# Retention and two feed-forward layers on one core: up products by Strassen's algorithm on pairs of token chunks, k and v rows of the longer prologue on ACT's DMA queue

## The reference

```python
for t in range(S):
    state = gamma * state + einsum('bhd,bhe->bhde', k[:, :, t], v[:, :, t])
    y[:, :, t] = scale * einsum('bhd,bhde->bhe', q[:, :, t], state)   # gamma[h] = 1 - 2^(-5-h)
x = y as (3072, 512)
h = x @ w_in;   g = h * cos(h);                       x = g @ w_out   # 512 -> 2048 -> 512
h = x @ w2_in;  g = where(h >= 1, h, where(h <= -1, 0, (h + 1)**2 / 4));  out = g @ w2_out
```

## Time and profile before

| what | value |
|---|---|
| median of 3 runs | 1165.73 us (1165.51 to 1165.99) |
| span of the profiled execution | 1163.8 us |
| granted TensorE clock, mean | 0.997 |
| PE busy | 1151.9 us, 99% |
| PE weight loads busy | 943.1 us, 81% |
| DVE / ACT / POOL busy | 556.8 / 380.4 / 132.4 us |
| instructions | 14906 |
| DMA | 74.57 MB, mean 64 GB/s |

### The profile page before, as it was taken

The page is one execution under the profiler, slowest core; times in us unless marked ns, Lnnn a source line. Parts: engine busy times, 40 slices in busy tenths (PEclk is TensorE's granted clock), DMA queues, the critical chain, the costliest instruction groups (busy, mean ns, idle before and its releaser), DMA issues.

```text
span 1163.8 us, 14906 instructions
## 1 busy us (share of the span) xinstructions
PE 1151.9 (99%) x5892; PEld 943.1 (81%) x5892; DVE 556.8 (48%) x836; ACT 380.4 (33%) x606; POOL 132.4 (11%) x113
## 2 busy tenths in 40 slices
PE   7999999999999999999999999999999999999998
PEld 5888888888888888788788888888888888888887
DVE  5555555556556555555554433433433433433433
ACT  2444332333333333323555322222222222222222
POOL 4445011001001010100354000000000000000000
PEclk8999999999999999999999999999999999999999
DMA  6433212022113112220452301001101001000100
GB/s 230 160 111 128 73 54 74 19 102 63 37 35 112 44 48 91 73 73 1 145 172 64 145 1 73 37 1 73 37 1 73 36 0 72 36 0 0 37 1 37
DMA packets 35481, 74.57 MB, mean 64 GB/s; under 512 B 3936, under 2 KB 4064, under 8 KB 33888
## 3 DMA queue, kind: packets, MB, share of 16 engines
q1 hardware_dynamic: 35424, 73.75, 18.7%
HBM read 54.86 MB, written 18.87 MB: 63 GB/s over the span
## 4 chain that ended last, share of the span: by engine, by line
PE 97%; DMA 1%; DVE 1%; SPq 0%; ACT 0%; issue 0%; DVEq 0%
PE up L378 45%; PE acc L401 23%; PE acc L403 22%; PE att L339 2%; PE att L318 2%; PE att L335 2%; PE att L359 1%; DMA raw<-in_w1u 0%; DMA q_sb<-in_q_t 0%; DVE x_lo L532 0%; PE acc L318 0%; PE att L354 0%; DVE am L471 0%; DVE x_lo L481 0%; DVE q_sb L461 0%
## 5 line engine op out<-in xcount | busy, mean ns | idle before, releaser
L378 PE MATMUL up<-x_hi,wu_hi 128*128 128x512 f32 x768 | 299.6, 390 | 1.1 <-DVE g_raw L514 1.1
L378 PE MATMUL up<-x_lo,wu_hi 128*128 128x512 f32 x768 | 298.8, 389 | 0.0
L378 PE MATMUL up<-x_hi,wu_lo 128*128 128x512 f32 x768 | 298.8, 389 | 0.0
L523 DVE SCALAR_TENSOR_TENSOR g_lo<-g_raw,g_hi 128x512 fp32r<-128x512 f32 x192 | 137.3, 715 | 181.9 <-ACT g_hi L608 181.9
L608 ACT ACTIVATE g_hi<-g_raw 128x512 fp32r<-128x512 f32 x192 | 121.3, 632 | 192.7 <-PE acc L403 108.8
L378 PEld LDWEIGHTS up<-x_hi,wu_hi 128*128 128x128 f32 x768 | 144.1, 188 | 32.8 <-DVE g_raw L514 2.5
L378 PEld LDWEIGHTS up<-x_hi,wu_lo 128*128 128x128 f32 x768 | 144.1, 188 | 30.0
L378 PEld LDWEIGHTS up<-x_lo,wu_hi 128*128 128x128 f32 x768 | 144.2, 188 | 29.7
L401 PE MATMUL acc<-g_hi,wd_hi 128*128 128x512 f32 x384 | 156.1, 406 | 0.0
L401 PE MATMUL acc<-g_hi,wd_lo 128*128 128x512 f32 x384 | 150.1, 391 | 0.0
L401 PE MATMUL acc<-g_lo,wd_hi 128*128 128x512 f32 x384 | 149.9, 390 | 0.0
(11 more groups left out here) (57 smaller groups left out, 899.5 us busy)
## 6 DMA issues: line engine op xcount, KB each, us to landing
q_sb<-in_q_t SPq DMA_DIRECT2D x24, 256.0 KB, 4.0
k_sb<-in_k_t SPq DMA_DIRECT2D x24, 256.0 KB, 4.0
x_hi_scratch<-x_hi SPq DMA_DIRECT2D x24, 256.0 KB, 3.0
x_lo_scratch<-x_lo SPq DMA_DIRECT2D x24, 256.0 KB, 3.4
x_hi<-x_hi_scratch SPq DMA_DIRECT2D x6, 1024.0 KB, 4.8
x_lo<-x_lo_scratch SPq DMA_DIRECT2D x6, 1024.0 KB, 6.9
kn<-in_k_n SPq DMA_DIRECT2D x22, 256.0 KB, 2.9
v_sb<-in_v_n SPq DMA_DIRECT2D x20, 256.0 KB, 2.6
```

The source lines that it names most:

```text
L378: last = nc.tensor.matmul(up[j % 2][:, :], w[:, j, k, :], x[:, par, k, :], start=(k == 0 and x is x_hi and w is wu_hi), stop=(k == KT - 1 ...
L523: nc.vector.scalar_tensor_tensor(out=g_lo[:, s, :], in0=g, scalar=2.0 if layer == 1 else 1.0, in1=g_hi[:, s, :].bitcast(F32), op0=ALU.mult ...
```

## The change

The up product of layer and chunk becomes one of a pair of chunks. X is cut into X11, X12 (k tiles 0, 1 and 2, 3 of the first chunk) and X21, X22 (the same of the second), W into four quarters by k half and by f half, and with Winograd's form of Strassen's algorithm seven products of half the depth take the place of eight. A quad q is the f tiles q and q + 8 of both chunks: its W quarters are 128 wide, it gives H11, H12, H21, H22. Three of four up banks hold the products of a quad; P6, P7 and P4 are added up in one bank, P1 and P2 in another, P5 and P3 in the third, and DVE adds what is between (`sum_u2`, `sum_u3`, `sum_h22`, `sum_h21`, `sum_h12`) from PSUM and SBUF.

A span is a pair of chunks in a layer: six spans of eight quads, then a tail. Down products of the first chunk of the pair go beside the quads (one of tile q - 1 behind P6, one of q - 1 + 8 behind P5), those of the second chunk's 16 tiles after the quads in the tail, 18 in all with the last two of the first. Their gates wait in SBUF (`late`).

Raw weights of up products are loaded again in each span, a quad at a time into two buffers; POOL makes four sums of 128 columns for each k tile (`t_sums`), ACT the high half of all seven blocks in one instruction of 896 columns (`t_high`), POOL the low half (`t_low`). The sums of X are made by POOL (512 columns, 8 a span), the splits of the 14 operand tiles by ACT and DVE. In layer 1 the multiplication with 1/(2 pi) goes from DVE to ACT (`turns`).

The prologue has eight units of retention, with all q, k, v and row-form k of them in buffers of their own but one; SP issues q and k, ACT issues the rows of k and v of units 0 to 6 as its first instructions. The other sixteen units lie in the tails of spans 0 and 1, in one block each of outputs, outer products and the scores of the next unit, with one down product (two behind the last but one) between blocks. The last four units have no outer products. Layer 1's result is stored and read as one float32 tensor. All loops over chunks are written out. Down results leave PSUM by copies on ACT (`rows_first`, `rows_second`), except the last two of the program, on DVE.

```diff
-        def walk(eng, body):
...
-                    elif (layer, place) != (2, "last"):
-                        up_product(blk + 1, 1 - par, layer, "middle", j + LEAD - FT)
-                    if not opening:
-                        retention(blk, layer, place, j)
-                    down_product(blk, layer, place, j)
...
-                dve.wait_ge(up_done, n + 1)
-                if layer == 1:
-                    nc.vector.tensor_scalar(g.bitcast(I32), h, TURNS, None, ALU.mult).then_inc(turns_done, 1)
...
+PRODUCTS = ["p1", "p6", "p2", "p7", "p5", "p4", "p3"]
+BLOCK = {"p1": 0, "p7": 1, "p2": 2, "p3": 3, "p5": 4, "p6": 5, "p4": 6}
+W11, W12, W21, W22, T1, T2, T4 = range(7)
...
+SPLITS = [("p1", 0, X11), ("p1", 1, X11 + 1), ("p2", 0, X12), ("p2", 1, X12 + 1), ("p7", 0, X11), ("p7", 1, X11 + 1),
+          ("p4", 0, X22), ("p6", 0, SUM2), ("p5", 0, X21), ("p3", 0, X12),
+          ("p4", 1, X22 + 1), ("p6", 1, SUM2 + 1), ("p5", 1, X21 + 1), ("p3", 1, X12 + 1)]
+NS = len(SPLITS)
+SUMS_BEFORE = {4: 1, 5: 2, 7: 3, 8: 4, 9: 5, 11: 6, 12: 7, 13: 8}
+NSUM = 8
...
+DOWN = [(1, f) for q in range(QUADS - 1) for f in (q, q + QUADS)]
+LATE = [f for q in range(QUADS) for f in (q, q + QUADS)]
+TAIL = [(1, QUADS - 1), (2, LATE[0]), (2, LATE[1]), (1, FT - 1)] + [(2, f) for f in LATE[2:]]
+DOWN += TAIL
+ND = len(DOWN)
...
+        def quad_banks(s, q):
+            return [up_banks(s)[(3 * q + i) % 4] for i in range(3)]
+        def unit_banks(u):
+            if u < AHEAD:
+                return banks[0:4] if u % 2 == 0 else banks[4:8]
+            return early_banks(u // AHEAD - 1)
...
+            def load_rows(u):
+                first = u < AHEAD
+                if not first and u % AHEAD >= 1:
+                    sp.wait_ge(y_done, u)
+                    sp.wait_ge(outer_done, min(u, UNITS - KT))
+                sp.dma_start(unit_kn(u), heads(k_n[u])).then_inc(kn_in_first[u] if first else kn_in, 16)
+                sp.dma_start(unit_v(u), heads(v_n[u])).then_inc(v_in_first[u] if first else v_in, 16)
+            def load_raw(n):
+                layer, q = n // (QUADS * PAIRS), n % QUADS
+                if n >= 2:
+                    sp.wait_ge(product_done["p3"], n - 1)
+                if n % QUADS == 1 and n // QUADS in (1, 2):
+                    sp.wait_ge(y_done, AHEAD * (n // QUADS + 1))
+                    sp.wait_ge(outer_done, min(AHEAD * (n // QUADS + 1), UNITS - KT))
+                for kt in range(2):
+                    sp.dma_start(raw[n % 2][:, kt, 1, 0:4, :], up_input[layer][q, kt]).then_inc(raw_in[n % 2][kt], 16)
...
+            for s in range(SPANS):
+                for q in range(QUADS):
+                    n = QUADS * s + q + 1
+                    if n < QUADS * SPANS:
+                        load_raw(n)
+                    if q == 0 and s:
+                        store_rows(s - 1, 2)
+                    if s == 0 and q + 1 < QUADS:
+                        load_wd(0, q + 1)
+                u = AHEAD * (s + 1)
+                if s < PAIRS - 1:
+                    load_columns(u)
+                    load_rows(u)
+                    load_columns(u + 1)
+                elif s + 1 < SPANS:
+                    load_x2(s + 1, 0)
+                store_rows(s, 1)
+                if s < PAIRS - 1:
+                    load_rows(u + 1)
+                    for i in range(2, AHEAD):
+                        load_columns(u + i)
+                        load_rows(u + i)
+                elif s + 1 < SPANS:
+                    load_x2(s + 1, 1)
+                if s == PAIRS - 1:
+                    for q in range(QUADS):
+                        load_wd(1, q)
...
+            def product(s, q, name):
+                n = QUADS * s + q
+                i = BLOCK[name]
+                bank_1, bank_2, bank_3 = quad_banks(s, q)
+                to = {"p1": bank_1, "p2": bank_1, "p6": bank_2, "p7": bank_2, "p4": bank_2,
+                      "p5": bank_3, "p3": bank_3}[name]
+                if q == 0:
+                    pe.wait_ge(xlo_done, NS * s + max(m for m in range(NS) if SPLITS[m][0] == name) + 1)
+                if name == "p1" and q >= 2:
+                    pe.wait_ge(h12_done, n - 1)
+                if name == "p6" and q >= 1:
+                    pe.wait_ge(g_done, 4 * (n - 1) + 1)
+                if name == "p5" and q >= 1:
+                    pe.wait_ge(h21_done, n)
+                if name == "p2":
+                    pe.wait_ge(p1_copied, n + 1)
+                if name == "p7":
+                    pe.wait_ge(u2_done, n + 1)
+                if name == "p4":
+                    pe.wait_ge(u3_done, n + 1)
+                if name == "p3":
+                    pe.wait_ge(h22_done, n + 1)
+                w = tw[n % 2]
+                for kt in range(2):
+                    if name == "p1":
+                        pe.wait_ge(tlo_done, 2 * n + kt + 1)
+                    opens = name in ("p1", "p6", "p5") and kt == 0
+                    nc.tensor.matmul(to[:, :], w[:, kt, 0, i, :], x_hi[:, i, kt, :], start=opens, stop=False,
+                                     skip_group_check=True)
+                    nc.tensor.matmul(to[:, :], w[:, kt, 0, i, :], x_lo[:, i, kt, :], start=False, stop=False,
+                                     skip_group_check=True)
+                    last = nc.tensor.matmul(to[:, :], w[:, kt, 1, i, :], x_hi[:, i, kt, :], start=False, stop=kt == 1,
+                                            skip_group_check=True)
+                last.then_inc(product_done[name], 1)
...
+            for u in range(AHEAD):
+                outputs(u)
+                outer(u)
+                if u + 2 < AHEAD:
+                    scores(u + 2)
+            for s in range(SPANS):
+                if s == 0:
+                    pe.wait_ge(masked, 2 * (AHEAD - 1))
+                    pe.wait_ge(x_copied, AHEAD - 1)
+                    pe.wait_ge(state_done, 2 * (AHEAD - 1))
+                elif s < PAIRS:
+                    pe.wait_ge(masked, 2 * AHEAD * (s + 1))
+                    pe.wait_ge(x_copied, AHEAD * (s + 1))
+                    pe.wait_ge(state_done, 2 * min(AHEAD * (s + 1), UNITS - KT))
+                else:
+                    pe.wait_ge(rows1_done, 4 * s)
+                for q in range(QUADS):
+                    product(s, q, "p1")
+                    product(s, q, "p6")
+                    if q:
+                        down(s, 1, q - 1)
+                    product(s, q, "p2")
+                    product(s, q, "p7")
+                    product(s, q, "p5")
+                    if q:
+                        down(s, 1, q - 1 + QUADS)
+                    product(s, q, "p4")
+                    product(s, q, "p3")
+                tail = list(TAIL)
+                if s < PAIRS - 1:
+                    u = AHEAD * (s + 1)
+                    for _ in range(5):
+                        down(s, *tail.pop(0))
+                    scores(u)
+                    down(s, *tail.pop(0))
+                    for i in range(AHEAD):
+                        outputs(u + i)
+                        outer(u + i)
+                        if i + 1 < AHEAD:
+                            scores(u + i + 1)
+                            for _ in range(BETWEEN[i]):
+                                down(s, *tail.pop(0))
+                for item in tail:
+                    down(s, *item)
...
+            def sum_u2(s, q):
+                n = QUADS * s + q
+                dve.wait_ge(p1_copied, n + 1)
+                dve.wait_ge(product_done["p6"], n + 1)
+                nc.vector.tensor_tensor(work[:, U2, :], quad_banks(s, q)[1][:, :], work[:, S1, :],
+                                        ALU.add).then_inc(u2_done, 1)
+            def sum_u3(s, q):
+                n = QUADS * s + q
+                dve.wait_ge(product_done["p7"], n + 1)
+                nc.vector.tensor_tensor(work[:, U3, :], quad_banks(s, q)[1][:, :], work[:, S1, :],
+                                        ALU.add).then_inc(u3_done, 1)
...
+            def finish(s, q):
+                angle(s, q, 2)
+                if q == QUADS - 1:
+                    gate_low(s, *TAIL[1])
+                angle(s, q, 3)
+            def quad(s, q):
+                if q:
+                    finish(s, q - 1)
+                sum_u2(s, q)
+                if q:
+                    gate(s, q - 1, 2)
+                    gate(s, q - 1, 3)
+                    gate_low(s, 1, q - 1 + QUADS)
+                angle(s, q, 0)
+                sum_u3(s, q)
+                gate(s, q, 0)
+                sum_h22(s, q)
+                gate_low(s, 1, q)
+                angle(s, q, 1)
+                gate(s, q, 1)
+                sum_h21(s, q)
+                sum_h12(s, q)
...
+            def turns(s, q, k):
+                n = QUADS * s + q
+                if s >= PAIRS:
+                    return
+                if k == 0:
+                    act.wait_ge(product_done["p2"], n + 1)
```

(84 more changed lines are left out.)

1000 lines of the change are left out of this document (538 added, 462 removed).

## The result

The change made the kernel slower: 1208.67 us median of 4 runs (1204.12 to 1209.53) beside 1165.62 for the kernel before on the same chip, ratio 1.0367 (1.0348 to 1.0386). Forecast were 1138, range 1106 to 1163. The profiled span is 1207.7 us, 71.4 more than the 1136.3 of the sum; mean granted clock 0.971, before 0.997.

A forecast was written before the change was run, and what follows sets the result against it. PE was taken as the bound, busy 1151.9 of 1163.8 us. 1163.8 - 65.3 - 26.0 + 25.8 + 23 + 9 + 6 = 1136.3 us of span, with 1.9 outside it forecast 1138; range 1106 to 1163.

The forecast's parts named there:

- the lock: POOL instruction reading SBUF blocks DVE instruction with two SBUF inputs; one block a layer 1 quad, 0.35 us a tail unit.
- What goes: Up products on PE: 2016 matmuls instead of 2304, 288 x 0.2267 = 65.3 us saved in full.
- the 65 and 26 us: Predicted savings on PE: 65.3 us from fewer up matmuls, 26.0 us from retention units as blocks in the tails.
- The longer prologue: Eight retention units ahead of the products: up work begins in effect at 53.3 instead of 27.5, +25.8 us.
- The ring: Prologue loop of mask, outputs and outer, state update, next mask: 34.5 us from the first mask to the last.
- The quads: Layer 1 quads 16.0 us against PE's 14.96, +23 us over 24 quads, bounds 0 and 60; layer 2 quads 14.96.
- The tails: Behind the spans: +9 us for 14 retention rounds, +6 for six span ends, rows copies and wd_high at the layer change.
- Matmul spacing: On PE, throughout: distance from one matmul to the next still 0.2267 us.
- (d): Accumulating two products in one bank puts gaps between matmuls, so 288 fewer save nothing; 1200 us, chance 0.02.
- (a): Clean quads: neither lock nor chain costs PE anything, layer 1 quads every 15 us; 1110 us, chance 0.19.
- (b): Prologue and retention tails longer: half clock +12 us, late v in 14 rounds +7; 1157 us, chance 0.15.
- (c): Narrow POOL sums don't shrink, weights come late; slower than before from 1.03 us a sum, 1263 at 1.29; chance 0.06.

The follow-up runs named there:

- c3: c2 with the rows of k and v back on SP's queue and, in the prologue, the state updated behind a unit's sums and splits; 1123.16 us, 0.9649.
- after: The changed kernel itself, as measured and profiled, against the kernel before; 1208.67 us, 1.0367.
- c1: Changed kernel with early t_high, wd_low on DVE, earlier prologue splits, new weight addresses, and g_lo behind the next mask in retention tails; 1145.80 us, 0.9833.
- c2: c1 with X's eight sums on DVE, prologue splits back behind the units, two t_low held there until the seventh unit's mask; 1137.63 us, 0.9777.
- early t_high: Changed kernel with ACT's two t_high of a quad issued one step earlier, ahead of a g_hi and of sine 0; 1182.86 us, 1.0137.
- e2: Changed kernel with tb, half_one and probe allocated behind the up weights, which then start at 128 modulo 256 bytes; 1198.65 us, 1.0303.
- the pad in the old order: Changed kernel with an unused 128-byte tile ahead of the weight tiles, which then start at 128 modulo 256 bytes; 1207.71 us, one run.

## Why the prediction was wrong

The step that failed is the lock's reach. The prediction had it as one block a quad (+23 us), 0.35 us a unit in the tails and a part of 2 us in the prologue; it also lay over wd_low in span 0, over the sums of X in the tails and over the first splits. Beside it the start was mis-sized (+25.8 us said, +42.4 found) and the matmul spacing was taken over from other addresses.

**What goes: right.** 2016 up matmuls, and with weights at the old alignment each at the old price. c3 shows that the 65 and 26 us were there to be had: 41 us are left after all that the new order costs.

**The longer prologue: failed (+16.6).** The first up matmul was put at 50 and came at 59.84, past the 56 that the prediction had named as a sign against it. Three terms. The rows of k and v on ACT's queue: the start of the first mask was put at 9.4 and came at 12.79, 3.4 later. The ring from first to last mask was put at 34.5 and took 43.0 (12.79 to 55.74). Part of it is the lock; in after, the fourth split, which stands ahead of a mask, began just behind a t_low:

```profile
40.65 2.07 POOL L926 TENSOR_TENSOR tw<-raw,tw 128x896 fp32r<-128x896 f32 x1 [14.60 <-ACT tw L724]
...
40.71 2.57 DVE L533 TENSOR_TENSOR x_lo<-work,x_hi 128x512 fp32r<-128x512 f32 x1
```

That is 2.57 us for 0.69, 1.9 more. With the new addresses, in the same prologue, the split began at 39.45, the t_low at 39.60, and the split took 0.69. Another part is half clock: the outputs of a unit took 1.98 us where they take 1.09 in c3, and from mask to state update two rounds took 5.81 and 6.41 us, 4.22 each with the new addresses, 3.8 together. That kernel's ring, at a granted clock of 0.96 from 12 to 52 us (0.70 in after), took 37.0 us. So of the 8.5 us some 2.5 are missing from the ring's sum at nearly full clock too, 1.9 are the lock and 3.8 the clock; the prediction had 2 for the last two. The third term is PE's wait in the first quad: 3.3 predicted, 10.1 found. After's timeline:

```profile
59.28 0.63 PE L370 MATMUL bank<-late 128*64 128x64 f32 x16
...
60.17 4.65 POOL L943 TENSOR_TENSOR work<-work 128x512 f32<-128x512 f32 x3 [1.39 <-ACT work L709]
60.86 10.54 DVE L533 TENSOR_TENSOR x_lo<-work,x_hi 128x512 fp32r<-128x512 f32 x10
...
64.78 0.90 POOL L916 TENSOR_TENSOR raw<-raw 128x128 f32<-128x128 f32 x1
```

The prediction counted the splits that stand behind POOL's last sums; ten stand behind the last unit, in order, and beside POOL's sums of X and of weights each takes 1.05 us instead of 0.69. For these ten the lock had no price of its own.

**The quads: right in mechanism and size in spans 1 and 2, failed in span 0 (+15.4).** "The second t_low lies over g_lo of (1,q)" is what the rows show, and 15.79 us a quad was given as 16.0. But span 0 has wd_high and wd_low in each quad besides; 2.8 us of POOL that read SBUF, right behind t_low, were in no term. The prediction named the place of one block ("g_lo starts 1.6 later and takes angle 1 with it") and did not ask what POOL does next. Over the 24 quads 36 us were lost; the upper bound of 60 holds that, but 2.5 a quad doesn't hold span 0's 3.2 (18.18 less 14.96).

**The tails: failed (+34.0).** "0.35 for the lock" a unit and "+6" for six ends. POOL's sums of X (48, 40 of them in the tails, 1.26 us each at the least, mean 1533 ns), each with both operands in SBUF, block DVE's splits and g_lo beside them. In the first tail of after:

```profile
282.85 10.18 POOL L943 TENSOR_TENSOR work<-work 128x512 f32<-128x512 f32 x6
...
285.08 1.75 DVE L574 SCALAR_TENSOR_TENSOR g_lo<-late,g_hi 128x512 fp32r<-128x512 f32 x1
286.76 3.48 DVE L533 TENSOR_TENSOR x_lo<-work,x_hi 128x512 fp32r<-128x512 f32 x2
...
294.50 0.50 PE L430 MATMUL bank<-g_hi,wd_hi 128*128 128x512 f32 x1 [4.21 <-DVE g_lo L574]
```

Without POOL's reads for the low halves tails 0 and 1 took 90.3 and 87.6 us; c1 had 88.0 and 87.4, and c2, with the sums off POOL, 84.2 and 83.8, where 86.2 and 83.6 were expected. The sum of the round was off too: its terms (2.0 to 1.4) give 6.73 and not 6.95, which is 3 us in 14 rounds the other way. At the change of layers the sums add up with a load; after's timeline:

```profile
659.29 0.94 SPq L239 DMA_DIRECT2D wd_raw<-in_w2d  x2
...
664.21 1.06 ACT L732 ACTIVATE wd_hi<-wd_raw 128x1024 fp32r<-128x1024 f32 x1 [4.26 <-DMA wd_raw<-in_w2d]
...
666.56 0.50 PE L430 MATMUL bank<-g_hi,wd_hi 128*128 128x512 f32 x1 [2.42 <-DVE g_lo L574]
...
667.18 10.96 POOL L943 TENSOR_TENSOR work<-work 128x512 f32<-128x512 f32 x7 [5.07 <-DVE x_lo L533]
...
667.63 1.77 DVE L533 TENSOR_TENSOR x_lo<-work,x_hi 128x512 fp32r<-128x512 f32 x1
```

ACT stood 4.26 us for the DMA with the next g_hi queued behind, which the prediction had named without a price. Then seven sums on POOL, a split at 1.77 and PE waiting. With wd_low on DVE and its first load ahead of the stores tail 2 fell to 58.8, with the new addresses, the early t_high and the order of c1 to 55.4, with the sums off POOL to 50.6: what had been expected (50.0).

**Matmul spacing: failed (+6.4 of layer 2's 8.4).** "Matmul spacing still 0.2267" was taken over from a kernel with other addresses. Rival (d) had put a changed spacing to accumulation in the banks; that fell (14.96 in e2 with the same accumulation).

**The rivals.** (a) named 14.3 to 15 us a quad as its sign; it is the picture of c1 to c3, not of the change. (b) had the half clock in the prologue, at 12; its late v, at 7, is 0.3 us in PE's waits. The prologue and the tails lost 50.6; of the half clock 3.8 are read above, and most came otherwise. (c), POOL's narrow sum, is refuted at its price: 0.45 to 0.46 us alone, forecast 0.42. Slower was right with another mechanism: POOL's low halves cost some 50 to 55 us, while PE's own waits on POOL were 3.7 us; the rows show them blocking DVE. No rival had the lock as the mechanism that turns the change slower, though the rows with 1.77 and 1.81 stood there; a chance of 0.09 for slower was too small for a change that takes POOL from 132 to some 600 us beside a DVE whose inputs had moved from PSUM to SBUF.

**Open.** (1 - 0.971) / 0.5 of 1207.7 is 70 us at half clock (1.2 of 2.4 GHz), against 7 before; what they cost in all is known for two rounds alone. Seven kernels have the change's prologue. In three of them (after, early t_high, the pad in the old order) the fourth split was held (2.40 to 2.57 us), and the ring took 42.8 to 44.1 us; in the other four it took 0.69 and the ring 37.0 to 39.8. Which of the two comes hangs on some tenths of a microsecond. The granted clock from 12 to 52 us was 0.70, 0.83 and 0.70 in the three, 0.96, 0.96, 0.79 and 0.79 in the four; why it differs from one kernel to the next, no run here shows.

## What to carry to other kernels

Before work is given to an idle POOL, list for each stage which DVE instructions read two SBUF operands, and charge every POOL instruction that reads SBUF, up to its full length, to the one it will lie over, in the prologue and the tails as much as in the loop, one after the other where POOL has two in a row. A bound engine that is relieved soon isn't the bound: then the order of each engine within the round decides (two instructions a quad issued earlier were worth 27 us, with not one less). And DMAs of a second queue are not free: they take their share from the ones that are waited for.

## What the runs showed of the hardware

- The start address of the weight tile sets the matmul's spacing: 14.96 us for 66 matmuls at 128 modulo 256 bytes, 15.24 to 15.29 at 0 and 192; 128 and 0 were each tried in two regions of SBUF, 192 in one.
- A DVE instruction held by POOL is shown as a long instruction, not as a wait: 2.18 us for 0.69, with no idle time in the bracket. The waits of the profile then name DVE, and POOL has 1.0 and 2.7 us in PE's list where some 50 to 55 us went with its low halves.
- POOL's own 128-column sum took 0.45 to 0.46 us alone and had a mean of 597 to 680 ns in after, held in turn by DVE.
- Half clock came behind many long waits of PE and not behind all: after the 4.21 us wait that ended at 294.50 the matmuls start 0.43 us apart from 295.7 to 298.6, while after one of 2.50 us that ended at 57.29 and one of 2.11 at 88.25 the granted clock stayed full for over 9 us.
- The same order of work gave starts that lie 7 us apart: in seven kernels with one prologue the first up matmul came at 54.52 to 61.69 us.
